# The last product of the later two thirds as seven gated block products, with split weights kept in DRAM

## The reference

```
x   = attention(q, k, v)              # 4 x 8 heads, softmax within chunks of 64
x   = ((x @ w_a) * (x @ w_b)) @ w_out                  # d_ff 1536
p   = domain_probs / (domain_probs.sum(-1) + 1e-9)     # 4 experts
out = sum over e of p[:, e] * (relu(x @ w1[e]) @ w2[e])   # w1 512x1024, w2 1024x512
```

## Time and profile before

| | |
|---|---|
| median of 3 runs | 1219.96 us (1219.95 to 1220.03) |
| the profiled execution | 1219.97 us, span 1217.9 us, granted clock 0.999 |
| busy share of the span | PE 99%, PEld 93%, DVE 67%, ACT 44% |
| DMA | 98.73 MB, read 92.84 MB and written 4.72 MB, 81 GB/s over the span |

### The profile page before, as it was taken

One profiled execution on the slowest core, in us unless ns is written; L12 is line 12 of the kernel. 1 busy time (PEld: TensorE's weight loads), 2 busy tenths in 40 slices (PEclk: granted clock), 3 DMA queues, 4 the chain that ended last, 5 costly groups with the idle time before them and its releaser, 6 DMA issues.

```text
span 1217.9 us, 18367 instructions
## 1 busy us (share of the span) xinstructions
PE 1210.2 (99%) x7527; PEld 1128.0 (93%) x7527; DVE 820.7 (67%) x1222; ACT 538.8 (44%) x939; POOL 0.7 (0%) x6
## 2 busy tenths in 40 slices
PE   8999999999999999999999999999999999999998
PEld 8999998888889899999888888989999999999997
DVE  5786476666676877647766677687765666666664
ACT  5554363443445455526343344536542633333332
POOL 0000000000000000000000000000000000000000
PEclk9999999999999999999999999999999999999999
DMA  7123132222211222213222212123221121122211
GB/s 262 36 69 96 44 130 92 68 93 96 96 64 49 89 96 70 87 52 104 92 92 96 95 69 67 66 87 105 69 83 57 69 69 70 70 70 69 69 36 52
DMA packets 27875, 98.73 MB, mean 81 GB/s; under 512 B 3216, under 2 KB 3216, under 8 KB 21648
## 3 DMA queue, kind: packets, MB, share of 16 engines
q1 hardware_dynamic: 27792, 97.57, 23.3%
HBM read 92.84 MB, written 4.72 MB: 80 GB/s over the span
## 4 chain that ended last, share of the span: by engine, by line
PE 95%; DVE 3%; ACT 1%; issue 1%; ACTq 0%; DVEq 0%
PE ps L333 31%; PE ps L335 30%; PE ps L334 30%; PE ps L361 1%; PE ps L342 1%; PE ps L369 1%; PE ps L350 1%; DVE x L969 1%; DVE w L969 0%; DVE h L1204 0%; PE ps L405 0%; ACT x L628 0%; DVE xraw_b L1230 0%; DVE xraw L1228 0%; DVE xraw L1367 0%
## 5 line engine op out<-in xcount | busy, mean ns | idle before, releaser
L333 PE MATMUL ps<-w,h 128*128 128x512 f32 x576 | 227.4, 395 | 0.5 <-DVE h L1204 0.5
L333 PE MATMUL ps<-x,w 128*128 128x384 f32 x672 | 225.0, 335 | 0.3
L335 PE MATMUL ps<-x,w 128*128 128x384 f32 x672 | 224.9, 335 | 0.0
L334 PE MATMUL ps<-x,w 128*128 128x384 f32 x672 | 224.6, 334 | 0.0
L335 PE MATMUL ps<-w,h 128*128 128x512 f32 x576 | 224.4, 390 | 0.0
L334 PE MATMUL ps<-w,h 128*128 128x512 f32 x576 | 224.3, 389 | 0.0
L628 ACT ACTIVATE ps<-ps 128x384 f32<-128x384 f32 x160 | 75.9, 477 | 286.1 <-PE ps L335 284.9
L1218 DVE SCALAR_TENSOR_TENSOR acc<-ps,pw,acc 128x512 f32<-128x512 f32 x126 | 94.4, 749 | 116.1 <-PE ps L335 115.5
L333 PE MATMUL ps<-x,wab 128*128 128x384 f32 x504 | 169.1, 335 | 0.0
L335 PE MATMUL ps<-x,wab 128*128 128x384 f32 x504 | 168.4, 334 | 0.0
L334 PE MATMUL ps<-x,wab 128*128 128x384 f32 x504 | 168.4, 334 | 0.0
(11 more groups left out here) (114 smaller groups left out, 1603.8 us busy)
## 6 DMA issues: line engine op xcount, KB each, us to landing
raw<-in_w SPq DMA_DIRECT2D x48, 1024.0 KB, 4.8
raw<-in_wab SPq DMA_DIRECT2D x36, 512.0 KB, 4.7
raw<-in_wo SPq DMA_DIRECT2D x36, 256.0 KB, 2.7
out<-acc SPq DMA_DIRECT2D x18, 256.0 KB, 2.0
q_sb<-in_q SPq DMA_DIRECT2D x12, 256.0 KB, 5.2
k_sb<-in_k SPq DMA_DIRECT2D x12, 256.0 KB, 5.4
v_sb<-in_v SPq DMA_DIRECT2D x12, 256.0 KB, 5.5
late<-in_q SPq DMA_DIRECT2D x4, 256.0 KB, 8.5
```

The costliest lines, as they stand in the source:

```text
L333: pe.matmul(dst, stat(HI), mov(HI), start=first, stop=False, skip_group_check=True)
L334: pe.matmul(dst, stat(HI), mov(LO), start=False, stop=False, skip_group_check=True)
L335: return pe.matmul(dst, stat(LO), mov(HI), start=False, stop=last, skip_group_check=True)
```

## The change

The first third keeps its windows (`first_phase`), with additions. The later two thirds get new ones (`later_phase`, `make_h`, `make_out`).

- **First third, kept weights.** SP stores the split parts of each window's w1 (3 DMAs, 128 x 7168 float32 in all) and w2 (three DMAs of its four blocks' parts). The four sums of w2's blocks, which the seven products need, are made by DVE (`sum_w2`, four operations of 512 elements), rounded by ACT (`round_wt`), their rests by DVE (`low_wt`), and stored (2 DMAs, 128 x 4096). The buffers `three` and `lone` are used again in the next window, so `sum_w2` waits until the stores of the last one have landed; likewise the splits of w1 and w2 wait for their stores.
- **Later thirds, loads.** The split parts come straight from DRAM: 3 DMAs for w1 and 2 for w2 per window, 7.3 MB; no sum or split of w1 or w2 remains there. The token weights of an expert are loaded onto all partitions (`pb`).
- **Later thirds, products.** `make_h` makes the same seven products in another order, with attention between them. h is gated before the product: `gate` takes relu and multiplies by the token weight in one DVE operation of 768 elements. Four sums of the gated h follow (`hs_sum`), ACT rounds seven blocks, DVE makes seven rests, and `make_out` makes seven block products of 12 matmuls of 384 columns, with features on partitions. Six DVE additions of 768 elements per window (`add_to`) take them into `acc_t` and `c2`; the fifth and sixth product pile onto banks that ACT seeds with one copy (`x_seed`), which waits for the addition "a4". In window 7 DVE folds the shared parts together. The host puts the output's blocks in place by transposing.
- **Memory.** `w1s` lies over `raw`, `tsum` and `lone`; `three` and `pb` lie in the region of `x`.

The diff, cut to its core:

```diff
+            def first_windows():
+                load_w2(0)
+                for w in range(PH):
+                    t = TILES + w
+                    sp.wait_ge(w1_lo, 3 * w + 3)
+                    if w < PH - 1:
+                        load_w1(w + 1)
...
+                    for n in range(3):
+                        sp.dma_start(kept_w1[w, :, w1_part(n)], w1[:, w1_part(n)].bitcast(F32)).then_inc(w1_kept, 16)
+                    if w < TILES:
...
+                        sp.wait_ge(scored, t - 1)
+                        load_qk(t)
+                        sp.wait_ge(attended, t - 1)
+                        load_v(t)
+                    sp.wait_ge(w2_lo, 2 * w + 2)
+                    for b, at in ((0, 1), (1, 5), (3, 6)):
+                        sp.dma_start(kept_w2[w, :, at], w2[:, :, b, :].bitcast(F32)).then_inc(w2_kept, 16)
+                    if w < PH - 1:
+                        sp.wait_ge(wt_sum, 4 * w + 4)
+                        load_w2(w + 1)
...
+                    for u in ((w,) if w < 6 else (6, 7) if w == 6 else ()):
+                        sp.wait_ge(wt_lo, 2 * u + 2)
+                        sp.dma_start(kept_w2[u, :, 2:5], three[:, :].bitcast(F32)).then_inc(wt_kept, 16)
+                        sp.dma_start(kept_w2[u, :, 0], lone[:, :].bitcast(F32)).then_inc(wt_kept, 16)
...
+            def make_out(T, w):
+                def block(n, first_bank, first):
+                    pe.wait_ge(hw_lo, hw_count(T, w, H_ORDER[n]))
+                    for s in range(2):
+                        for kt in range(2):
+                            at = kt * 256 + s * P
+                            last = product(ps[:, first_bank + s, 0:N], lambda part: w2s[:, n, part, at:at + P],
+                                           lambda part: hw[:, H_PLACE[n], part, kt, :], first and kt == 0, kt == 1)
+                        last.then_inc(O_MADE[n], 1)
...
+                block(0, 2, True)
+                block(1, 0, True)
+                block(2, 4, True)
+                pe.wait_ge(gated, 4 * V + 4)
+                block(3, 6, True)
+                pe.wait_ge(w2s_in[1], 16 * V + 16)
+                pe.wait_ge(x_seed, V + 1)
+                block(4, 2, False)
+                block(5, 0, False)
+                if T < NTH - 1 and w < TILES:
+                    pe.wait_ge(cleared, w + 1)
+                    score(t, 6, True)
+                pe.wait_ge(evac, evac_no(T, w, "a5"))
+                block(6, 4, False)
...
+                act.wait_ge(o1_made, 2 * V + 2)
+                act.wait_ge(evac, evac_no(T, w, "a4"))
+                copy(block_of(2), block_of(0)).then_inc(x_seed, 1)
```

More of the change, by code:

```diff
@@ L38, with build @@
 PLACES = ((2, 1, 0, 3), (0, 1, 2, 3))
+H_ORDER = (A22, A11, S1, S3, S2, A12, S4)
+H_PLACE = (3, 0, 2, 4, 6, 5, 1)
+H11, H22, H21, H12 = range(4)
+G11, G4, G5, G53 = range(4)
+G7, GU = range(2)
+EVAC = ("a4", "a7", "a5", "u", "c11", "a53")
 AB_X = (XA11, XS3, XS2, XA12, XS1, XA22, XS4)
 AB_W = (B11, T3, T2, B21, T1, T4, B22)
-def build(nc, q, k, v, wab_in, wo_in, w1_in, w2_in, probs, out):
+def build(nc, q, k, v, wab_in, wo_in, w1_in, w2_in, probs, out, out_t):
     D = BLK
@@ L1270, in run_phase @@
                     for n in range(4):
-                        sum_w1(T, w + 1, n)
-                elif ahead:
+                        sum_w1(w + 1, n)
+                else:
+                    for n in range(4):
+                        sum_ab(1, 0, n)
+                add_out(w, 0)
+                if not last:
+                    split_w1(w + 1, 0)
+                else:
+                    low_ab(1, 0, 0)
+                    low_sum(1, XS1)
+                if w == 6:
+                    low_wt(6, 0)
+                    low_wt(6, 1)
@@ new lines, in first_phase @@
+                if w == 0:
+                    sum_w2(0)
+                add_out(w, 1)
+                if not last:
+                    split_w1(w + 1, 1)
+                else:
+                    low_sum(1, XS2)
+                    low_sum(1, XS3)
+                add_out(w, 2)
+                if not last:
+                    split_w1(w + 1, 2)
+                else:
+                    low_sum(1, XS4)
+                    low_ab(1, 0, 1)
+                add_out(w, 3)
+                if last:
+                    low_ab(1, 0, 2)
+                    low_ab(1, 0, 3)
@@ L1302, in run_phase @@
-                add_out(T, w, 5)
+                dve.wait_ge(o3_made, 2 * V + 2)
+                if w == PH - 1:
+                    dve.wait_ge(folded, 6 * T)
+                add_to(acc_t[:, G53], 4, "a53").then_inc(evac, 1)
+                if last:
+                    low_sum(T + 1, XA12)
+                    sum_x(T + 1, XS4)
+                    for a in (XS1, XS2, XS3, XS4):
+                        low_sum(T + 1, a)
+                    for n in range(1, 7):
+                        low_ab(T + 1, 0, n)
```

876 lines of the change are left out of this document (625 added, 251 removed).

## The result

The changed kernel takes 1264.56 us (median of 4 runs, 1262.51 to 1266.76) against 1219.95 (median of 4): a ratio of 1.0367, 95% interval 1.0347 to 1.0386. It is slower by 44.6 us; forecast were 24, within a range up to 1266. The sign was right, and so was the order of the two largest terms; the size was not. The profiled execution is the fastest of the four: 1262.51, span 1260.7 against 1217.9.

What follows compares the result with a forecast made beforehand. PE bounds the kernel, busy 99%; S is PE's start of a window. 27.8 - 6.9 - 24 - 3.3 - 12 - 2.9 - 3.4 = -24.7: 1219.97 becomes 1244.7, said as 1244, range 1217 to 1266.

Steps and rivals of the forecast that it cites:

- slow stores: First third: stores slower than loads, q and k cost 52 us at 300 GB/s, kernel 1272; chance 0.1.
- What PE saves: Later thirds, 16 windows: 72 matmuls of 512 columns become 84 of 384, saving 1.74 us each, 27.8 in all.
- the seed: Later windows, fifth block product: PE waits 0.4 us for ACT's copy; 6.9 us over 16 windows, bounds 0 and 14.
- The fourth rival: Later windows: seed and rests late by 0.9 us in each, since DVE's chain is tight; kernel 1251; chance 0.1.
- q and k: First third, `score`, windows 1 to 5: loads queued behind 6.82 MB, PE waits 4.8 us each, 24 in all; bounds 0, 52.
- The first rival: First third: q and k land before PE needs them, 24 us goes; kernel 1220 down to 1210; chance 0.2.
- the second (300 GB/s): First third: stores slower than loads, q and k cost 52 us instead of 24, kernel 1272; chance 0.1.
- The clock: Granted clock halves behind long PE waits at 1.7 us each; two longest of seven waits counted, 3.4 us; bounds 0, 12.
- the third rival: Clock falls behind every long PE wait: 12 us in place of 3.4, kernel 1253; chance 0.15.
- Windows 6 and 7 of the first third: Window 7's sums of w2 wait for window 6's stores; last `add_out` late, PE loses 3.3 us; bounds 0, 7.
- From the middle to the last third: DVE's longer tail in window 7 delays both weight blocks: waits 4.6 and 6.6 us, 12 with S4's 0.7; bounds 6, 16.
- The end: Last window: S4 late, DVE's last addition and a store of 1.5 times the size; 2.9 us lost, bounds 1, 4.

Runs made afterwards that it cites:

- the scratch matmuls: Changed kernel with 90 small bf16 matmuls ahead of `score` in windows 1 to 5 of the first third: 1256.52 us, ratio 1.0296.
- the same mistake made on a smaller scale in window 6: With q, k, v issued first, window 6's sums of w2 go ahead of the next w1; w2's load for window 7 behind stores 1223.11 us, ahead 1218.61.

## Why the prediction was right in sign and short in size

The forecast's steps against the difference of the spans, 42.8 us; windows 7 are counted with the stretch that they open. The loss forecast for the span was 24.7. The measured 1264.56 lies within the range, but 1.4 us from its end, and that end was set for another case, slow stores, which did not happen: in this the range was lucky.

- **What PE saves, and the seed: right.** Forecast were 1.74 less 0.43, 1.31 a window; measured 1.30 in windows 1 to 5 of the middle third and 1.38 in the last third (30.97 against 29.59). The seed's wait is 0.22; the fifth product starts at S + 23.26 (1069.77 - 1046.51), forecast was S + 23.35. The other 0.14 of the 0.36 that the second part takes beyond 84 x 0.1736 are two gaps of 0.08, at its start and behind the first matmul of the fifth product; so a seed that waits less than forecast and gaps that were not forecast nearly cancel. The fourth rival (0.9 late each window) did not happen.
- **q and k: right mechanism, 24 forecast, 32.4 measured.** The waits were 5.2 in windows 3 and 4, near the 4.8 forecast, and 6.6 to 8.2 in the others. Three things were short: the rate, 371 to 381 GB/s from S to the end of the wait in place of 400 (17.05 us become 17.9 and more); the first store's issue, at S - 0.0 in window 1 in place of S - 1.0 (in the others it is at S - 1.1); and the bytes. From the first store's issue to k's landing pass 21.0 us in windows 3 and 4, 22.3 to 23.0 in 1, 2 and 5, all at 367 to 370 GB/s: 7.7 MB there, 8.2 to 8.5 here, so in 1, 2 and 5 more of the stores behind k was moved ahead of k's landing. The forecast held the queue to be strictly in order. Why it lets more pass in these windows was not tried and is open. The first rival (q and k in time) is excluded, the second (300 GB/s) too. The 600 GB/s of the first rival's condition was worked out too high: 6.82 MB in the 12.3 us that its terms leave are 554.
- **The clock: the step that failed.** The forecast took 3.4, a fall behind the two longest waits. The clock fell in all five waits for k. The five windows lost 41.4 us, of which 32.4 are waits; 9.0 are `score` and matmuls behind them, nearly all by the half clock, since the scratch matmuls gave 8.0 back (8.4 in the profiled windows). A stretch that begins within the wait also takes in `score`, `turn_p` and the first dense matmuls. This is the third rival, held at 0.15, and its price of 1.7 each was about right (8.0 / 5 = 1.6). At the start of the last third one fall has two parts: ahead of the second wait the half clock costs nothing, the wait is only shorter (4.7 in place of the 6.6 forecast, while the first product takes twice its 2.08); behind it the second product takes 1.8 us more, and PE does not wait again. No run tried whether that can be gained back in this order; with the tail reordered it cannot, since PE waits at the fifth product anyway.
- **Windows 6 and 7 of the first third: 3.3 forecast, 6.3 measured**, 5.2 in window 7 and 1.1 in the pairs behind. The last addition was forecast at S + 36.1 and came at S + 37.9 (445.51 - 407.64); before it came at S + 32.4 (399.64 - 367.21, PE's start of that window), not S + 32.9. What was missed is that ACT's split of the next w1 waits for the stores of the last one (4.24 us), and the rounding of the sums 6 stands behind that split.
- **From the middle to the last third: right but for the clock.** 12 less the saving of that window, 10.7, against 12.6; 1.8 of the 1.9 are the second product at half clock. The rest of the first weight block was forecast for S + 35.0 and is ready at S + 35.1 (870.25 - 835.16); PE got the second at S + 44.1, forecast S + 43.8. Counting the list of an engine that is busy 98% of the time holds over 35 us.
- **The end: 2.9 less 1.3 forecast, 2.3 measured.** DVE's last addition ends at S + 32.6 as worked out (1256.64 - 1224.05); the last store landed 3.7 us behind its issue at S + 36.3, where the forecast left it about 2.2, and the span ends at S + 36.7, forecast S + 34.9. The four stores were issued within 2.3 us, before each had the queue to itself; whether the size or the crowd makes them slower was not tried. That the loss is only 0.7 over the forecast is because what it was measured against, S + 32.0, was worked out too low as well: before, the span ends at S + 34.4, less 1.3 that is S + 33.1.

In sum: q and k 8.4 more than forecast, the clock behind these waits 5.6, windows 6 and 7 3.0, the middle to the last third 1.9 (the clock as well), the end 0.7, less 0.4 for PE's saving and 1.0 at the start: 18.2 on top of 24.7, 42.9.

## What to carry to other kernels

When a change puts stores into a queue that also brings operands, count the bytes ahead of each load whose user can't wait, and issue those loads first: here one place in SP's list was 43 us of 44.6, and the same mistake made on a smaller scale in window 6 cost 4.5 (1223.11 against 1218.61). On an engine without idle time, moving work within its list mostly moves the wait (4.6 us earlier at the second product, 2.3 left at the end); take work away, or to where the engine idles. A wait of TensorE of 5.2 to 8.2 us among dense matmuls cost 1.6 us on top for the clock here; it costs nothing where TensorE has to wait for another engine behind it anyway.

## What the runs showed of the hardware that was not expected

- The granted clock fell to 0.50 while PE still stood in its wait (full until 219.00, 0.50 from 221.00 in a wait from 215.9 to 224.2), and rose again behind 1.83 us of small matmuls and 1.4 us of dense ones. Scratch matmuls on 128 columns during the wait, 90 in 5.2 us, kept it at 1.00. In the last third's first pair, with the scratch matmuls, it fell 0.8 us behind a wait of 2.07 us, and 1.5 us were lost; without them, at the same place, it did not fall behind a wait of 1.68 us.
- Stores of 0.5 to 1.6 MB and loads on one queue together moved 371 to 381 GB/s over 20 us, with a DMA share of 0.98 to 1.00, within the range of loads alone.
- One queue was worked off nearly but not strictly in order: 7.3 MB were issued up to k, and 7.7 to 8.5 MB had been moved when it landed.
- SP's issues take longer when much is queued: three stores of w1's parts took 4.13 us to issue, the three of w2's parts behind them 7.30 (209.24 to 216.54), against 0.33 for the first store of the window.
